# Two narrower token pairs of the MLP made equal: 480 and 480 tokens a tile in place of 496 and 464

## The reference

```
scores = scale * np.matmul(z, z.transpose(0, 2, 1))      # z: (2, 3008, 64), scale = 1/3008
attn = np.maximum(scores, 0.0) ** 2
out = np.matmul(attn, v)                                 # v: (2, 3008, 256)
x = (u * out).reshape(6016, 256)

h = x @ w_in                                             # first MLP: 256 -> 2048 -> 256
x = (h - np.tanh(h)) @ w_out

gate = 1.0 / (1.0 + np.exp(-(x @ w_gate)))               # second MLP: 256 -> 1536 -> 256
return (gate * (x @ w_val)) @ w_out2
```

## Time and profile before

| | us |
|---|---|
| median of 3 runs | 1496.04 |
| lowest and highest | 1495.21, 1496.99 |
| the profiled execution, its own time | 1496.93 |
| its span, first to last instruction | 1495.1 |
| TensorE busy (share of the span) | 1489.9 (100%) |
| TensorE's weight loads busy | 1256.0 (84%) |
| VectorE busy | 1135.4 (76%) |
| ScalarE busy | 949.5 (64%) |
| granted TensorE clock, share of full speed | 1.00 |

### The profile page before, as it was taken

The page is one execution under the profiler, slowest core; times in us unless marked ns, Lnnn a source line. Parts: engine busy times, 40 slices in busy tenths (PEclk is TensorE's granted clock), DMA queues, the critical chain, the costliest instruction groups (busy, mean ns, idle before and its releaser), DMA issues.

```text
span 1495.1 us, 21893 instructions
## 1 busy us (share of the span) xinstructions
PE 1489.9 (100%) x8796; PEld 1256.0 (84%) x8796; DVE 1135.4 (76%) x1416; ACT 949.5 (64%) x1285; POOL 0.5 (0%) x5
## 2 busy tenths in 40 slices
PE   9999999999999999999999999999999999999999
PEld 8888888888888888888888888888888888888888
DVE  8999988999987787777676777666666676666656
ACT  8677767777766666666666666655556555555554
POOL 0000000000000000000000000000000000000000
PEclk9999999999999999999999999999999999999999
DMA  4444422254434345453535456453636454554452
GB/s 141 139 162 151 152 81 86 89 213 159 159 121 172 116 154 186 155 196 131 211 138 186 155 177 234 172 191 127 246 127 218 156 199 173 190 186 185 151 194 89
DMA packets 37365, 241.79 MB, mean 162 GB/s; under 512 B 3600, under 2 KB 8720, under 8 KB 23952
## 3 DMA queue, kind: packets, MB, share of 16 engines
q1 hardware_dynamic: 37120, 240.16, 44.1%
q10 hardware_dynamic: 144, 0.24, 0.0%
HBM read 196.21 MB, written 44.17 MB: 161 GB/s over the span
## 4 chain that ended last, share of the span: by engine, by line
PE 100%; ACT 0%; DVE 0%; issue 0%; DVEq 0%
PE acc L563 25%; PE hidden L632 13%; PE hidden L635 13%; PE hidden L630 13%; PE acc L524 10%; PE acc L525 10%; PE acc L523 10%; PE hidden L550 6%; PE acc L729 0%; PE acc L743 0%; PE acc L736 0%; DVE x_out L1294 0%; ACT part_hi L935 0%; ACT h L932 0%; DVE part_lo L1165 0%
## 5 line engine op out<-in xcount | busy, mean ns | idle before, releaser
L1046 DVE TENSOR_TENSOR part_lo<-h,part_hi 128x1024 fp32r<-128x1024 f32 (+5 forms) x317 | 375.2, 1184 | 82.3 <-ACT part_hi L882 49.9
L874 ACT ACTIVATE snap<-hidden 128x512 f32<-128x512 f32 (+2 forms) x360 | 211.8, 588 | 249.3 <-PE hidden L635 249.0
L632 PE MATMUL hidden<-region 128*128 128x512 f32 (+2 forms) x840 | 323.6, 385 | 0.0
L630 PE MATMUL hidden<-region 128*128 128x512 f32 (+2 forms) x840 | 323.6, 385 | 0.0
L635 PE MATMUL hidden<-region 128*128 128x512 f32 (+2 forms) x840 | 323.5, 385 | 0.0
L563 PE MATMUL acc<-part_hi,region 64*128 64x512 f32 (+1 forms) x2256 | 286.1, 383 | 0.7 <-ACT part_hi L935 0.7
L1136 DVE TENSOR_TENSOR h<-hidden,snap 128x512 f32<-128x512 f32 (+2 forms) x252 | 170.7, 678 | 142.5 <-ACT snap L874 115.7
L525 PE MATMUL acc<-part_hi,region 128*128 128x512 f32 (+2 forms) x664 | 256.1, 386 | 0.0
L524 PE MATMUL acc<-part_lo,region 128*128 128x512 f32 (+2 forms) x664 | 256.0, 386 | 0.0
L523 PE MATMUL acc<-part_hi,region 128*128 128x512 f32 (+2 forms) x664 | 255.9, 385 | 0.0
L563 PEld LDWEIGHTS acc<-part_hi,region 64*128 64x128 f32 x2256 | 216.1, 184 | 39.4 <-issue 1.1
(11 more groups left out here) (68 smaller groups left out, 1149.9 us busy)
## 6 DMA issues: line engine op xcount, KB each, us to landing
region<-ready SPq DMA_DIRECT2D x33, 2304.0 KB, 8.8
region<-ready SPq DMA_DIRECT2D x51, 1408.0 KB, 6.1
ready<-region SPq DMA_DIRECT2D x6, 2304.0 KB, 7.4
ready<-region SPq DMA_DIRECT2D x8, 1408.0 KB, 6.0
xs<-x_out SPq DMA_DIRECT2D x18, 512.0 KB, 6.0
x_in<-xs SPq DMA_DIRECT2D x16, 512.0 KB, 8.1
snap<-vP SPq DMA_DIRECT2D x24, 256.0 KB, 2.7
u_in<-uT SPq DMA_DIRECT2D x10, 512.0 KB, 5.2
```

The source lines that it names most:

```text
L630: pe.matmul(dst, weights[0], x[0], start=i < 3, stop=False, skip_group_check=True)
L632: pe.matmul(dst, weights[0], x[1], start=False, stop=False, skip_group_check=True)
L874: act.activation(snap[:, g % 2, i, 0:w], hidden[:, CHAIN[g % 2], 0:w], ACT.Copy).then_inc(s_snap, 1)
L1046: return ve.tensor_tensor(dst, whole, hi.bitcast(F32), ALU.subtract)
```

## The change

One line: the last two pairs get 480 tokens a tile each. `PAIR_WIDTHS` also sets which tokens a pair holds, so that pair 5 and pair 11 begin 32 tokens earlier. Every instruction, wait and DMA stays in its place and number; the ones of pairs 4, 5, 10 and 11 have another size.

```diff
-PAIR_WIDTHS = (512, 512, 512, 512, 496, 464)
+PAIR_WIDTHS = (512, 512, 512, 512, 480, 480)
 assert len(PAIR_WIDTHS) == PAIRS and 2 * sum(PAIR_WIDTHS) == ALL and max(PAIR_WIDTHS) <= TOK
```

## The result

| | us |
|---|---|
| before, median of 18 runs | 1495.71 (1494.90 to 1497.37) |
| changed, median of 18 runs | 1498.66 (1498.05 to 1499.60) |
| ratio, 95% interval | 1.0018 (1.0012 to 1.0025) |
| profiled execution, before and changed | 1496.93 and 1498.65 |
| span, before and changed | 1495.1 and 1496.8 |

The medians differ by 2.95 us; the ratio of 1.0018 stands for 2.7 us (1.8 to 3.7 by its interval). The forecast was -0.8 with a range up to 1497.4, so both sign and range were wrong.

A forecast was written before the change was run, and what follows sets the result against it. The prediction took TensorE's matmul pitch to bound the kernel. Its terms, -0.88 for layer 2, 0.0 for layer 1 and +0.05 for the end, gave -0.8 against the median 1496.04, so 1495.2 us, range 1492.7 to 1497.4.

The forecast's parts named there:

- What bounds the kernel: Whole kernel: TensorE's matmul count times pitch sets the time; no other engine or DMA limits it over any long stretch.
- Part 1: Layer 2, pairs 10 and 11: 480 at 0.21333 us pitch, 169.84 to 168.96 us, -0.9 us.
- the line: Pitch straight in width through 512 and layer 2's 496, 0.000417 us a column plus a fixed part; 0.21333 at 480.
- the weight load as a floor: At 464, the 0.188 us load plus about 0.021 us needed keeps pitch up; at 480, 0.025 us left, so not binding.
- the slow rhythm: Slower pitch after a late weight load, 0.0034 us over at 496 in layer 1; 512 leaves it after seven matmuls.
- Part 2: Layer 1, pairs 4 and 5: late load again, 480 stays slow at 0.2161 us, 0.0 us; -2.0 if it leaves.
- Parts 3 and 4: Kernel end, wider pair 11: +0.05 us; VectorE and ScalarE stay hidden in the four pairs, they and DMAs cost nothing.
- The offset to the median: Profiled execution, 1496.93 us, lay 0.9 above the median 1496.04, perhaps by chance; the sum was taken from the median.
- A: All 480-wide pairs leave the slower pitch, 0.21333 us: sum -2.85, so 1493.2 us; chance 0.27.
- B's slow end: 480 at the slower pitch, 0.2161 us, in layer 2 as well: 1497.4 us; a third of 0.19.
- C: All four 480-wide pairs at 0.2181 us after a late weight load, 0.0048 excess: +4.3, so 1500.4 us; chance 0.07.
- The formula of the Trainium skill: Every matmul: warm distance N/2.4 ns plus 2.5, straight in N, making the change worth 0.

The follow-up runs named there:

- e7: Kernel before with 480 and 480 in layer 2 only, layer 1 keeping 496 and 464; 1497.80 us, ratio 1.0011.
- m1: Changed kernel with a ladder of bare matmuls, 512 to 448 columns, weight blocks of 128, 112 and 64, ahead of its first score; adds some 0.9 ms.
- e8: Kernel before with 480 and 480 in layer 1 only, layer 2 keeping 496 and 464; 1496.35 us, ratio 1.0003.
- m2: Changed kernel with bare matmuls ahead of its first score: 24 of 512 columns, then another width, in part with a wait mid-stretch; no total time given.
- e6: Kernel before with two blocks of second swapped and ScalarE's second snapshot ahead of the high parts in layer 1; 1495.02 us, ratio 0.9992.
- e9: Kernel before with widths 510 four times, 496 and 472, the same columns in sum; 1499.68 us, ratio 1.0020.
- e5: Kernel before with widths 512 twice and 496 four times, and two blocks of second swapped in layer 1; 1500.99 us, ratio 1.0028.
- e3: Kernel before with the first two blocks of second swapped in the first unit of pairs 1 to 5, layer 1; 1496.83 us, ratio 0.9997.

## Why the prediction was wrong

**What bounds the kernel: right.** TensorE's pitch decides, waits and DMAs didn't move, VectorE and ScalarE stayed hidden.

**Part 1, layer 2 on the line, -0.9 us: wrong, and this is the step that failed.** I drew the line through 512 and 496, two points at the top of their stairs, and read it at 480. The measured +1.8 (e7: +1.8) is 792 x 0.0033 = 2.6 above my figure. The step behind it was my reason for 464 being off the line, the weight load as a floor with room to spare at 480. It fell for 480 with m1, where 53 ns less of load left the pitch where it was and 13 ns less made it worse. That 464 came down to the line with a 64-column load fits a floor, 0.2100 with 112 columns does not, and why 464 lies where it does stays open. The claim that nothing sets the slow rhythm off in layer 2 was true for 496 and beside the point for 480, which is never at 0.2133 with a 128-column block.

**Part 2, layer 1, 0.0 us at 0.2161: the size nearly right (0.2167, +0.4; e8: +0.3), the reason wrong.** The load was late again, by 0.07 us, and the pitch was slow in both pairs. But it is slow there without a late load too. 0.2161 was the mean of two neighbours, one of them slowed by a late load; that it came near is luck. For 496 the reason was right, as m2 and e6 show; I carried it over to a width where it plays no part.

**Parts 3 and 4, the end and the other engines: right.** No loss or gain beyond 0.1 us shows; pitch alone accounts for 2.1 of the 2.95 us.

**The offset to the median: partly wrong.** I took the profiled execution of before as 0.9 above its median. With 18 runs it was 1.2 above, and the changed one lay on its median, so that the profiles show 1.7 and the medians 2.95. The 0.85 us between the pitches and the medians are inside the interval (1.8 to 3.7), and I can't place them. Attention alone moves single executions by more: over the thirteen profiled ones of the full kernel the first MLP matmul starts between 479.3 and 480.6 us. And the median of the kernel before went from 1495.71 to 1496.77 between groups of runs.

**The rivals.** A (all on the line) is out. B's slow end, 480 slow in layer 2 as well, came nearest, with a time 1.3 us below the measured one: its pitch was 0.0006 low, 0.9 us. It had a third of 0.19, and it took 480 for a slow rhythm where the runs show the only one. C had one pitch in all four pairs, but set off by a late load, and 0.0048 over the line where it is 0.0033. The formula of the Trainium skill ("TensorE: Matmul & The Clock Gate", section "Back-to-back issue gap"), which that section gives for an isolated matmul and which is straight in the columns, also ends at no change; e9 measured +3.1 us where every straight line gives 0, so the measurement decides against it.

## What to carry to other kernels

Measure the pitch at the width itself before trading columns between tiles; two points make a line whatever lies between. With these operands the cost of a matmul goes up in steps of 16 columns at most widths from 472 to 512, so a tile wants to end on top of a stair that has a fast rhythm (512 and 496 here, not 480). And where TensorE shows no wait, look for weight loads that come even 10 ns behind the matmul before them: at 496 one such load, caused by one misplaced copy, cost 1.5% of the pitch until the width changed.

## What the runs showed of the hardware that I had not expected

- The pitch with 128 x 128 weight blocks moves in stairs at 14 of the 21 even widths from 472 to 512: 0.2267 us from 498 to 512 columns, 0.2200 from 482 to 496, 0.2133 from 472 to 478. Of the others 480 (0.2167) and 494 (0.2233) are slower than their stair, and 500 and 502 (0.2233) faster. Below 472 the stairs don't fit.
- 496 has two rhythms, 0.2200 and 0.2233, and 464 two, 0.2089 and 0.2100. At 496 the entry or one late load within the stretch decides which, and it lasts to the end of the stretch. 512 comes back by itself, behind the wait of m2 after seven matmuls.
- How late a load may be isn't settled. 11 ns ended the fast rhythm at 1239 us in e5, while one 61 ns late at 652 us in the same run did not, and one 63 ns late at 815 us in e3 did.
- The weight load takes 188 ns for 128 columns, 175 for 112, 135 for 64 and 108 for 32, so it isn't proportional to the columns: these four lie on 81 ns plus 0.83 ns a column. And at 512 the 64-column load made the pitch worse, 0.2300 in place of 0.2267.
- In attention, untouched by the change, the 448-wide tiles ran at one of two speeds in different executions, 0.1014 or 0.1033 us from start to start, in one (e8) with a change in the middle of a tile and back. The MLP's first matmul came at 480.3 us in one profile and 479.8 in the other.
